# One pair of heads ahead of the others in the first tile of an attention ramp

## The chip, the cores and the metric

The kernel runs on one core of one Trainium2 chip. The metric is the device time of one execution in microseconds, taken as the median of several runs.

## The reference, cut to what matters

Two batches, 8 heads, 768 positions, head size 64. Every query sees 4 sink keys at the start of the sequence and a window of 128 keys; two mixers follow, which hold most of the work and which the change does not touch.

```python
scores = q @ k.transpose(0, 1, 3, 2) / sqrt(64)
keep = (pos[None, :] < 4) | ((rel >= 0) & (rel < 128))   # rel = query - key
a = softmax(where(keep, scores, -1e9))                    # over the keys
x = (a @ v).transpose(0, 2, 1, 3).reshape(2, 768, 512)
# first mixer
u = x + (x^T @ U @ V)^T ; x = u + relu(u @ w_ch1) @ w_ch2
# second mixer, the same with relu between t1 and t2
```

## The kernel before, in words

The core works through one list, `plan`, that every engine walks in the same order; each engine does its own part of each step and waits on semaphores for the others. Attention goes by tiles T of 128 queries and, in each, by heads h; the unit u = 8T + h. For unit u the list holds ("scores", u), ("probsT", u - 2), ("pv", u - 4) for batch 0, and the steps that prepare tile T + 1 stand between them.

What is done to a unit: TensorE makes the scores, in three passes of split numbers (high query by high key, high by low, low by high); VectorE adds the mask and takes the minimum (`masked`, L1172); ScalarE takes the exponential (`probs`, L919); GpSimd copies the probabilities of the sinks into `p_sink` (L853); TensorE transposes the probabilities (L1463), which VectorE (even units) or ScalarE (odd ones) copies to `probs_T` (L1191, L986); TensorE multiplies by v (L1483).

What is done to a tile before its scores: q and k arrive in `q_nat` and `k_nat` (SyncE, `load_qk`, L684 and L686). ("qT", T) and ("kT", T) are four TensorE transposes each, one for every pair of heads (L1430). For T = 0, VectorE makes `q_hi` and `q_lo` from the transposed bank (L1115, L1117), ScalarE the high keys (L959, L960), VectorE the low ones (L574). For T = 1 to 5, ScalarE copies the transposed q and k to SBUF (L944, L953), VectorE casts the high parts (L1126, L1146, L1150) and **GpSimd subtracts for the low parts**: the queries in one step (L563, at "qsplit"), the keys in two, for the even heads (L574, at "ksplit") and for the odd ones (L574, at "ksplit_odd"). Scores 8 (tile 1, head 0) wait for the first of these and scores 9 for the second.

`k_hi` and `k_lo` have three slots of keys for each pair and head of the pair, with the four sink keys behind each slot, and are zeroed at the start: `k_hi` by VectorE (L1089), `k_lo` by GpSimd (L794), each in two steps. GpSimd also makes the identity (L789, L791), zeroes the masks and `sink_raw`, which lies in `o_stage` (L797, L798), and builds four masks with 14 selects (L806), all at its start; masks 2, 3 and then 0 and 1 are used by tiles 0, 1, 2 and 3. SyncE loads the sink values with eight small transfers once `sink_raw` is zeroed, and copies them twice more; VectorE casts them at ("scores", 8) (L1106).

The steps in order for the first units, before: unit 0 is qT(0), kT(0), the splits, qT(1), scores 0; unit 1 scores 1; unit 2 kT(1), qsplit(1), scores 2, probsT 0; unit 3 scores 3, probsT 1; unit 4 scores 4, pv 0, probsT 2; unit 5 ksplit(1), scores 5, pv 1, probsT 3; unit 6 ksplit_odd(1), scores 6 and so on; unit 8 qT(2), scores 8, pv 4, probsT 6; unit 9 scores 9. `keep_busy` issues transposes of the identity into an unused bank (L1415): 8 before qT(0), 6 before qT(1), 2 before scores 0.

Of the kernel before, what the change touches and what calls it, by code (L numbers as in the profile page):

```python
# [5 lines left out]
def attention_then_two_mixers(  # L6
# [58 lines left out]
    def attention(b):  # L65
# [4 lines left out]
        for u in range(lo, hi + LAG_V):  # L70
            T, h = divmod(u, H)
            now, scores, turned, probsT, pv, behind = [], [], [], [], [], []
            if u == 0:
                now += [("qT", T), ("kT", T), ("qsplit", T), ("ksplit", T)]
# [4 lines left out]
            if u < hi and T + 1 < NTILES:  # L79
                (turned if b else now).extend([("qT", T + 1)] if h == 0 else  # L80
                                              [("kT", T + 1), ("qsplit", T + 1)] if h == (2, 3)[b] else [])
                if h == (4 if 0 < T < NQ else 5):
                    (behind if b else now).append(("ksplit", T + 1))
                if h == (6, 7)[b]:
                    now.append(("ksplit_odd", T + 1))
# [96 lines left out]
    BUSY_BEFORE = {("qT", 0): 8, ("qT", 1): 6, ("scores", 0): 2}  # L182
# [132 lines left out]
    with ExitStack() as ctx:  # L315
# [136 lines left out]
        k_first_high = sem("k_first_high")  # L452
        ksinks_high = sem("ksinks_high")
# [82 lines left out]
        def key_parts(k_pad, T):  # L536

            turned = k_full if T else by_pair(tp_banks[tp_bank_of["kT", 0]])
            for e in range(2):
                rows = slice(e * D, (e + 1) * D)  # L540
                src = turned[rows, :, :]
                yield (src, k_pad[rows, :, e, T % 3, 0:P],
# [6 lines left out]
        def queries_split(T):  # L549

            return T + 1 if T < NQ else 2 * (T + 1) - NQ
# [14 lines left out]
        def key_low(eng, wait, T, e):  # L566
# [3 lines left out]
            steps = ((3, 2), (1, 0)) if T == 0 else ((1, 0),)  # L570
            done = (keys_split(T - 1) if T else 0) + e * len(steps)
            for to, of in steps:
                wait(k_split, done)
                eng.tensor_tensor(low[to], low[of], high[to].bitcast(f32), ALU.subtract).then_inc(k_split, 1)  # L574
                done += 1
            wait(k_split, done)

        def keys_split(T):

            return sum(4 if t % NQ == 0 else 2 for t in range(T + 1))  # L580
# [29 lines left out]
        def wait_drained(eng, s):  # L610

            kind, at = s
            if s == ("qT", 0):
                eng.wait_ge(q_split, 1)
# [62 lines left out]
        def _(sp):  # L677
# [43 lines left out]
            load_qk(0)  # L721
# [65 lines left out]
        def _(pool):  # L787
# [5 lines left out]
            for part in (slice(0, 3, 2), slice(1, 2)):  # L793
                nc.gpsimd.memset(k_lo[:, :, :, part, :].rearrange("p a b s k -> p (a b) s k").bitcast(f32), 0.0) \  # L794
                  .then_inc(klo_zeroed, 1)
                if part.start == 0:
                    nc.gpsimd.memset(masks[:, :, :], 0.0).then_inc(masks_built, 1)  # L797
                    nc.gpsimd.memset(sink_raw[0:HS], 0.0).then_inc(vsink_zeroed, 1)  # L798
# [11 lines left out]
            for m, own in MASKS:  # L810
# [9 lines left out]

            split = copied = 0
            for s in plan:
                if s == ("scores", H + 7):
# [81 lines left out]
        def _(act):  # L905
# [20 lines left out]
            for s in plan:  # L926
# [28 lines left out]
                elif s == ("ksplit", 0):  # L955
                    act.wait_ge(khi_zeroed, 2)
                    act.wait_ge(tp_ready, tp_at["kT", 0] + 1)
                    for src, dst, sinks, sink_dst in key_parts(k_hi, 0):
# [128 lines left out]
        def _(dve):  # L1087
            for part in (slice(0, 3, 2), slice(1, 2)):
                nc.vector.memset(k_hi[:, :, :, part, :].rearrange("p a b s k -> p (a b) s k").bitcast(f32), 0.0) \  # L1089
                  .then_inc(khi_zeroed, 1)  # L1090
# [12 lines left out]
            for s in plan:  # L1103
# [8 lines left out]
                if s == ("qsplit", 0):  # L1112
                    turned = by_pair(tp_banks[tp_bank_of["qT", 0]])
                    dve.wait_ge(tp_ready, tp_at["qT", 0] + 1)
                    nc.vector.tensor_scalar(q_hi[:, 0, :, :], turned, -SCALE, None, op0=ALU.mult).then_inc(q_high, 1)  # L1115
                    dve.wait_ge(q_high, 1)
# [579 lines left out]
```

## Time and profile before

| | us |
|---|---|
| median of 3 runs | 623.8 (623.78 to 624.27) |
| profiled execution, its own time | 624.31 |
| its span, first to last instruction | 622.3 |

The profile is of one execution. Times in its rows are microseconds from the start of the span, mean durations are in ns. The engines are PE (TensorE), PEld (its weight loads), DVE (VectorE), ACT (ScalarE), POOL (GpSimd) and SP (SyncE; SPq is its issue of transfers). "out<-in" names what an instruction writes and reads. An "x3" at the end of a row of the timeline means that so many instructions are merged in it. PEclk is the granted clock of TensorE as a share of 2.4 GHz.

### The profile page before, as it was taken

What the parts mean: (1) busy time and instruction counts of PE and PEld (TensorE: products, weight loads), DVE (VectorE), ACT (ScalarE), POOL (GpSimd) and SP (SyncE); (2) the same over time, 40 slices, a digit from 0 to 9 for tenths busy, and PEclk for the clock granted to TensorE, in tenths of its full rate; (3) what the DMA queues carried; (4) which work ended last, traced back from release to release, by engine and by line L of the source; (5) the groups of instructions that cost most, each with busy time, mean ns of one, the idle gap of its engine ahead of it and who ended that gap; (6) DMA issues with size and microseconds to landing.
All of it is one profiled execution on the core that took longest, in us unless ns stands there. A gap on an engine that the chain in (4) does not pass through costs nothing.

```text
span 622.3 us, 10353 instructions
## 1 busy us (share of the span) xinstructions
PE 613.0 (99%) x3462; PEld 554.3 (89%) x3462; DVE 350.1 (56%) x756; ACT 323.0 (52%) x728; POOL 402.5 (65%) x425
## 2 busy tenths in 40 slices
PE   8999999999999999999999999999999999999997
PEld 6899799999999989999999888899998888999986
DVE  6777655464464646866566621685766227665411
ACT  5677665655645555645445344554453437454321
POOL 7776488887978684656656654666575537566352
PEclk9999999999999999999999999999999999999999
DMA  8573345354335334333232333323323433421151
GB/s 162 124 168 82 89 109 131 102 120 120 85 102 168 88 105 132 84 102 86 75 112 86 119 96 100 111 83 93 94 84 119 137 101 85 152 85 41 47 163 72
DMA packets 88467, 65.59 MB, mean 105 GB/s; under 512 B 43040, under 2 KB 72480, under 8 KB 88416
## 3 DMA queue, kind: packets, MB, share of 16 engines
q1 hardware_dynamic: 88416, 64.95, 38.2%
q8 instruction: 28, 0.46, 0.3%
q14 instruction: 23, 0.19, 0.1%
HBM read 61.52 MB, written 3.15 MB: 104 GB/s over the span
## 4 chain that ended last, share of the span: by engine, by line
PE 92%; POOL 2%; DVE 2%; ACT 1%; issue 1%; DMA 1%; SPq 0%; DVEq 0%; ACTq 0%; POOLq 0%
PE bank L1666 34%; PE bank L1407 23%; PE bank L1632 11%; PE bank L1483 5%; PE bank L1453 4%; PE bank L1591 3%; PE bank L1536 3%; PE bank L1463 2%; PE bank L1430 2%; PE bank L1562 1%; POOL w_lo L899 1%; PE bank L1517 1%; PE bank L1658 1%; DMA k_nat<-in_k_dram 1%; DVE b_lo L1276 1%
## 5 line engine op out<-in xcount | busy, mean ns | idle before, releaser
L899 POOL TENSOR_TENSOR w_lo<-w_raw,w_hi 128x512 fp32r<-128x512 f32 (+1 forms) x158 | 210.6, 1340 | 136.0 <-ACT w_hi L935 135.0
L935 ACT ACTIVATE w_hi<-w_raw 128x512 fp32r<-128x512 f32 (+1 forms) x158 | 96.6, 618 | 54.0 <-PE bank L1666 35.9
L1666 PE MATMUL bank<-w_hi,hid_hi 128*128 128x512 f32 x216 | 86.4, 400 | 0.0
L1666 PE MATMUL bank<-w_hi,hid_lo 128*128 128x512 f32 x216 | 85.0, 394 | 0.0
L1666 PE MATMUL bank<-w_lo,hid_hi 128*128 128x512 f32 x216 | 84.8, 393 | 0.0
L919 ACT ACTIVATE probs<-masked,neg_max 128x264 f32<-128x264 f32 (+1 forms) x96 | 47.7, 497 | 59.6 <-DVE neg_max L1172 58.9
L1666 PE MATMUL bank<-w_hi,y_hid 128*128 128x512 f32 x216 | 71.0, 394 | 0.2
L1172 DVE CUSTOM_DVE_ANT_0 masked<-bank,masks 128x264 f32<-128x264 f32 (+1 forms) x96 | 38.8, 405 | 28.0 <-PE bank L1453 25.1
L1483 PE MATMUL bank<-v_nat,probs_T 128*128 128x64 f32 x352 | 50.6, 262 | 0.3 <-ACT probs_T L986 0.2
L1483 PEld LDWEIGHTS bank<-v_nat,probs_T 128*128 128x128 f32 x352 | 47.9, 190 | 1.6 <-ACT probs_T L986 0.9
L1666 PEld LDWEIGHTS bank<-w_hi,y_hid 128*128 128x128 f32 x216 | 40.5, 188 | 9.5 <-POOL w_lo L899 1.5
L1666 PEld LDWEIGHTS bank<-w_hi,hid_lo 128*128 128x128 f32 x216 | 40.5, 188 | 8.9
L1407 PE MATMUL bank<-b_hi,a_hi_even 128*128 128x384 f32 x140 | 47.2, 337 | 0.1
L1407 PE MATMUL bank<-b_hi,a_lo_even 128*128 128x384 f32 x140 | 47.1, 336 | 0.0
L1407 PE MATMUL bank<-b_hi,a_lo_odd 128*128 128x384 f32 x140 | 47.0, 336 | 0.0
L1407 PE MATMUL bank<-b_hi,a_hi_odd 128*128 128x384 f32 x140 | 47.0, 335 | 0.0
L1407 PE MATMUL bank<-b_lo,a_hi_even 128*128 128x384 f32 x140 | 46.9, 335 | 0.0
L1407 PE MATMUL bank<-b_lo,a_hi_odd 128*128 128x384 f32 x140 | 46.9, 335 | 0.0
L1666 PEld LDWEIGHTS bank<-w_lo,hid_hi 128*128 128x128 f32 x216 | 40.7, 188 | 6.7
L1666 PEld LDWEIGHTS bank<-w_hi,hid_hi 128*128 128x128 f32 x216 | 40.7, 189 | 6.6
L1632 PE MATMUL bank<-uT_hi,w_hi 128*128 128x384 f32 x128 | 45.4, 354 | 0.2 <-POOL w_lo L899 0.2
L1632 PE MATMUL bank<-uT_hi,w_lo 128*128 128x384 f32 x128 | 43.2, 338 | 0.0
(181 smaller groups left out, 1495.7 us busy)
## 6 DMA issues: line engine op xcount, KB each, us to landing
w_raw<-in_moe_w_ch_dram SPq DMA_DIRECT2D x144, 256.0 KB, 2.8
w_raw<-in_moe_w_ch_dram SPq DMA_DIRECT2D x20, 512.0 KB, 3.5
q_nat<-in_q_dram SPq DMA_DIRECT2D x12, 256.0 KB, 3.2
k_nat<-in_k_dram SPq DMA_DIRECT2D x12, 256.0 KB, 4.0
v_nat<-in_v_dram SPq DMA_DIRECT2D x12, 256.0 KB, 4.0
out_dram<-o_stage SPq DMA_DIRECT2D x11, 256.0 KB, 3.4
w_raw<-in_moe_w_tok_dram SPq DMA_DIRECT2D x6, 256.0 KB, 2.7
w_raw<-in_moe_w_tok_dram SPq DMA_DIRECT2D x8, 192.0 KB, 2.3
```

The lines of the kernel that those rows point to most:

```text
L899: nc.gpsimd.tensor_tensor(w_lo[:, split % NW, 0:n], w_raw[:, split % NR, 0:n], w_hi[:, split % NW, 0:n].bitcast(f32), ALU.subtract) \
L919: nc.scalar.activation(probs[:, u % 4, 0:n], masked[:, u % 3, 0:n], ACT.Exp, bias=neg_max[:, u % (2 * H):u % (2 * H) + 1], scale=-1.0, acc ...
L935: nc.scalar.activation(w_hi[:, split % NW, 0:n], w_raw[:, split % NR, 0:n], ACT.Copy) \
L1172: nc.vector.tensor_tensor_reduce(out=masked[:, u % 3, 0:n], in0=s_slots(u)[0][:, 0:n], in1=masks[:, mask_of(T), 0:n], scale=1.0, scalar=3. ...
L1407: last = mm(bank[:, 0:HALF], w[at % 2][:, a, k, :], u[:, b_part, k, :], start=(first and n == 0), stop=(n == 5), skip_group_check=True)
L1430: last = nc.tensor.transpose(qk_bank(s)[:, p * P:(p + 1) * P], nat[:, T % 2, p * P:(p + 1) * P], ident[:, :])
L1453: last = mm(bank[:, 0:width(T)], queries, keys(ks, T, h // 2, h % 2), start=(n == 0), stop=(n == len(passes) - 1))
L1483: last = mm(o_bank(T)[:, h * D:(h + 1) * D], probs_T[:, u % 2, j * P:(j + 1) * P], v_nat[:, tile % 3, h * D:(h + 1) * D], start=(h == 0 an ...
L1536: last = mm(m_tile(use)[:, :], w[:, slot, cols], x[:, t % 2, :], start=(t == 0 and n == 0), stop=(t == NQ - 1 and n == 2), skip_group_chec ...
L1591: last = mm(m_tile((s[:4], d))[:, 0:HALF], tok[:, g, rows], w[:, slot, 0:HALF], start=False, stop=(g == KG - 1 and n == 2), skip_group_che ...
L1632: last = mm(m_tile(use)[:, 0:HALF], w[:, slot, rows], u[:, kk, cols], start=(n == 0), stop=(n == 3 * KD - 1))
L1666: last = mm(m_tile(use)[:, :], stationary, w[:, slot, :], start=False, stop=(final and n == 2), skip_group_check=True)
```

## The change

Tile 0 is split into its first pair of heads and the other three. The first pair's q and k (64 KB each) are loaded by transfers of their own, turned by one transpose each into banks of their own (new steps q0T, k0T), and split (q0split, k0split); scores 0 follow. Then come qT(0) for the other three pairs, scores 1, kT(0), qsplit(0) and ksplit(0) for the three pairs, qT(1), scores 2. Scores 0 to 3 each wait for their own part. kT(1) and qsplit(1) stand in unit 3 instead of unit 2. The identity transposes are 5 before q0T, 3 before scores 0 and 4 before qT(1).

The key arrays are zeroed by slot: `k_lo` slot 0 and the sink columns of the other slots first, the rest later on GpSimd; `k_hi` slot 2 goes from VectorE to GpSimd. GpSimd builds only the first mask at its start (4 selects), then zeroes `sink_raw`, then the slots; mask 3 (4 selects) is built at the step ("kT", 1) and masks 0 and 1 (6 selects) at ("scores", 5), ahead of that unit's `p_sink` copy.

```diff
@@ -71,14 +71,17 @@
             if u == 0:
-                now += [("qT", T), ("kT", T), ("qsplit", T), ("ksplit", T)]
+                now += [("q0T",), ("k0T",), ("q0split",), ("k0split",)]
+                behind += [("qT", 0)]
+            elif u == 1:
+                behind += [("kT", 0), ("qsplit", 0), ("ksplit", 0), ("qT", 1)]
             sinks_after = u - (LAG_T if b else LAG_V)
...
             if u < hi and T + 1 < NTILES:
-                (turned if b else now).extend([("qT", T + 1)] if h == 0 else
-                                              [("kT", T + 1), ("qsplit", T + 1)] if h == (2, 3)[b] else [])
+                (turned if b else now).extend([("qT", T + 1)] if h == 0 and u else
+                                              [("kT", T + 1), ("qsplit", T + 1)] if h == (2 if 0 < T < NQ else 3) else [])
                 if h == (4 if 0 < T < NQ else 5):
@@ -179,7 +182,7 @@
-    BUSY_BEFORE = {("qT", 0): 8, ("qT", 1): 6, ("scores", 0): 2}
+    BUSY_BEFORE = {("q0T",): 5, ("scores", 0): 3, ("qT", 1): 4}
     first, second, prepared = attention(0), attention(1), preparation(1, 1)
@@ -533,12 +540,27 @@
-        def key_parts(k_pad, T):
-
-            turned = k_full if T else by_pair(tp_banks[tp_bank_of["kT", 0]])
+        FIRST_BANKS = (banks[7], banks[3])
+        first_pair, other_pairs = slice(0, 1), slice(1, PAIRS)
+
+        def first_key_parts(k_pad, pairs):
+
+            turned = FIRST_BANKS[1][:, 0:P].unsqueeze(1)
+            if pairs is other_pairs:
+                turned = by_pair(tp_banks[tp_bank_of["kT", 0]])[:, pairs, :]
+            count = pairs.stop - pairs.start
             for e in range(2):
...
                 src = turned[rows, :, :]
+                yield (src, k_pad[rows, pairs, e, 0, 0:P],
+                       src[:, :, 0:N_SINK].unsqueeze(2).broadcast_to([D, count, 3, N_SINK]),
+                       k_pad[rows, pairs, e, :, P:BLK])
+
+        def key_parts(k_pad, T):
+
+            for e in range(2):
+                rows = slice(e * D, (e + 1) * D)
+                src = k_full[rows, :, :]
                 yield (src, k_pad[rows, :, e, T % 3, 0:P],
@@ -548,7 +570,7 @@
-            return T + 1 if T < NQ else 2 * (T + 1) - NQ
+            return T + 2 if T < NQ else 2 * (T + 1) - NQ + 1
@@ -567,17 +589,14 @@
             low, high = list(key_parts(k_lo, T))[e], list(key_parts(k_hi, T))[e]
-            steps = ((3, 2), (1, 0)) if T == 0 else ((1, 0),)
-            done = (keys_split(T - 1) if T else 0) + e * len(steps)
-            for to, of in steps:
-                wait(k_split, done)
-                eng.tensor_tensor(low[to], low[of], high[to].bitcast(f32), ALU.subtract).then_inc(k_split, 1)
-                done += 1
+            done = keys_split(T - 1) + e
             wait(k_split, done)
+            eng.tensor_tensor(low[1], low[0], high[1].bitcast(f32), ALU.subtract).then_inc(k_split, 1)
+            wait(k_split, done + 1)
...
-            return sum(4 if t % NQ == 0 else 2 for t in range(T + 1))
+            return sum(8 if t == 0 else 4 if t == NQ else 2 for t in range(T + 1))
@@ -611,7 +630,7 @@
             if s == ("qT", 0):
-                eng.wait_ge(q_split, 1)
+                eng.wait_ge(q_split, queries_split(0))
             elif kind == "qT":
@@ -718,7 +737,12 @@
-            load_qk(0)
+            for nat, x, loaded in ((q_nat, q, first_loaded[0]), (k_nat, k, first_loaded[1])):
+                sp.dma_start(nat[:, 0, 0:P].rearrange("p (h d) -> p h d", h=2), heads(x, 0)[:, 0:2, :]) \
+                  .then_inc(loaded, 16)
+            for nat, x, loaded in ((q_nat, q, q_loaded[0]), (k_nat, k, k_loaded[0])):
+                sp.dma_start(nat[:, 0, P:DM].rearrange("p (h d) -> p h d", h=H - 2), heads(x, 0)[:, 2:H, :]) \
+                  .then_inc(loaded, 16)
             load_v(0)
@@ -790,12 +814,14 @@
                                     base=0, pattern=[[-1, P]], channel_multiplier=1).then_inc(ident_ready, 1)
-            for part in (slice(0, 3, 2), slice(1, 2)):
-                nc.gpsimd.memset(k_lo[:, :, :, part, :].rearrange("p a b s k -> p (a b) s k").bitcast(f32), 0.0) \
-                  .then_inc(klo_zeroed, 1)
-                if part.start == 0:
-                    nc.gpsimd.memset(masks[:, :, :], 0.0).then_inc(masks_built, 1)
-                    nc.gpsimd.memset(sink_raw[0:HS], 0.0).then_inc(vsink_zeroed, 1)
+
+            def zero(k_pad, slots, cols):
+                part = k_pad[:, :, :, slots, cols].rearrange("p a b s k -> p (a b) s k")
+                return nc.gpsimd.memset(part.bitcast(f32), 0.0)
+
+            zero(k_lo, slice(0, 1), slice(0, BLK)).then_inc(klo_zeroed, 1)
+            zero(k_lo, slice(1, 3), slice(P, BLK)).then_inc(klo_zeroed, 1)
+            nc.gpsimd.memset(masks[:, :, :], 0.0).then_inc(masks_built, 1)
             built = 1
@@ -807,7 +833,8 @@
-            for m, own in MASKS:
+            def build(m, own):
+
                 keep(m, own, P, 0, -1, 1)
@@ -818,8 +845,18 @@
+            build(*MASKS[0])
+            nc.gpsimd.memset(sink_raw[0:HS], 0.0).then_inc(vsink_zeroed, 1)
+            for slot in (1, 2):
+                zero(k_lo, slice(slot, slot + 1), slice(0, P)).then_inc(klo_zeroed, 1)
+            zero(k_hi, slice(2, 3), slice(0, P)).then_inc(k_last_zeroed, 1)
             split = copied = 0
             for s in plan:
+                if s == ("kT", 1):
+                    build(*MASKS[1])
+                elif s == ("scores", 5):
+                    for mask in MASKS[2:]:
+                        build(*mask)
                 if s == ("scores", H + 7):
@@ -952,10 +989,14 @@
                                          ACT.Copy).then_inc(k_copied, 1)
-                elif s == ("ksplit", 0):
-                    act.wait_ge(khi_zeroed, 2)
-                    act.wait_ge(tp_ready, tp_at["kT", 0] + 1)
-                    for src, dst, sinks, sink_dst in key_parts(k_hi, 0):
+                elif s in (("k0split",), ("ksplit", 0)):
+                    first = s == ("k0split",)
+                    if first:
+                        act.wait_ge(khi_zeroed, 2)
+                        act.wait_ge(first_turned, 2)
+                    else:
+                        act.wait_ge(tp_ready, tp_at["kT", 0] + 1)
+                    for src, dst, sinks, sink_dst in first_key_parts(k_hi, first_pair if first else other_pairs):
                         nc.scalar.activation(sink_dst, sinks, ACT.Copy)
@@ -1085,9 +1126,9 @@
         def _(dve):
-            for part in (slice(0, 3, 2), slice(1, 2)):
-                nc.vector.memset(k_hi[:, :, :, part, :].rearrange("p a b s k -> p (a b) s k").bitcast(f32), 0.0) \
-                  .then_inc(khi_zeroed, 1)
+            for slots, cols in ((slice(0, 1), slice(0, BLK)), (slice(1, 3), slice(P, BLK)), (slice(1, 2), slice(0, P))):
+                part = k_hi[:, :, :, slots, cols].rearrange("p a b s k -> p (a b) s k")
+                nc.vector.memset(part.bitcast(f32), 0.0).then_inc(khi_zeroed, 1)
@@ -1109,13 +1150,17 @@
                                             ALU.subtract).then_inc(vsink_split, 1)
-                if s == ("qsplit", 0):
-                    turned = by_pair(tp_banks[tp_bank_of["qT", 0]])
-                    dve.wait_ge(tp_ready, tp_at["qT", 0] + 1)
-                    nc.vector.tensor_scalar(q_hi[:, 0, :, :], turned, -SCALE, None, op0=ALU.mult).then_inc(q_high, 1)
-                    dve.wait_ge(q_high, 1)
-                    nc.vector.scalar_tensor_tensor(out=q_lo[:, 0, :, :], in0=turned, scalar=-SCALE,
-                                                   in1=q_hi[:, 0, :, :].bitcast(f32),
+                if s in (("q0split",), ("qsplit", 0)):
+                    if s == ("q0split",):
+                        pairs, turned, done = first_pair, FIRST_BANKS[0][:, 0:P].unsqueeze(1), q_first_high
+                        dve.wait_ge(first_turned, 1)
+                    else:
+                        pairs, turned, done = other_pairs, by_pair(tp_banks[tp_bank_of["qT", 0]])[:, 1:, :], q_high
+                        dve.wait_ge(tp_ready, tp_at["qT", 0] + 1)
+                    nc.vector.tensor_scalar(q_hi[:, 0, pairs, :], turned, -SCALE, None, op0=ALU.mult).then_inc(done, 1)
+                    dve.wait_ge(done, 1)
+                    nc.vector.scalar_tensor_tensor(out=q_lo[:, 0, pairs, :], in0=turned, scalar=-SCALE,
+                                                   in1=q_hi[:, 0, pairs, :].bitcast(f32),
                                                    op0=ALU.mult, op1=ALU.subtract).then_inc(q_split, 1)
@@ -1129,17 +1174,22 @@
                         moved.then_inc(q_moved, 1)
-                elif s == ("ksplit", 0):
+                elif s in (("k0split",), ("ksplit", 0)):
+                    pairs, made = (first_pair, 0) if s == ("k0split",) else (other_pairs, 2)
                     dve.wait_ge(klo_zeroed, 2)
-                    for e in range(2):
-                        dve.wait_ge(k_first_high, e + 1)
-                        key_low(nc.vector, lambda sem, n: None, 0, e)
+                    for e, (low, high) in enumerate(zip(first_key_parts(k_lo, pairs), first_key_parts(k_hi, pairs))):
+                        dve.wait_ge(k_first_high, made + e + 1)
+                        for to, of in ((3, 2), (1, 0)):
+                            nc.vector.tensor_tensor(low[to], low[of], high[to].bitcast(f32),
+                                                    ALU.subtract).then_inc(k_split, 1)
                 elif s[0] == "ksplit":
...
                     if T == 1:
-                        dve.wait_ge(khi_zeroed, 2)
+                        dve.wait_ge(khi_zeroed, 3)
+                    if T == 2:
+                        dve.wait_ge(k_last_zeroed, 1)
                     if T >= 2:
@@ -1418,7 +1468,12 @@
                     keep_busy(BUSY_BEFORE[s])
-                if s[0] in ("qT", "kT"):
+                if s in (("q0T",), ("k0T",)):
+                    n = int(s == ("k0T",))
+                    pe.wait_ge(first_loaded[n], 16)
+                    nc.tensor.transpose(FIRST_BANKS[n][:, 0:P], (q_nat, k_nat)[n][:, 0, 0:P], ident[:, :]) \
+                      .then_inc(first_turned, 1)
+                elif s[0] in ("qT", "kT"):
                     T = s[1]
@@ -1426,19 +1481,22 @@
                         tp_free(s)
-                    for p in range(PAIRS):
+                    for p in range(0 if T else 1, PAIRS):
                         last = nc.tensor.transpose(qk_bank(s)[:, p * P:(p + 1) * P],
...
                     T, h = divmod(u, H)
-                    if h == 0:
+                    if T == 0 and h < 4:
+                        pe.wait_ge(q_split, h // 2 + 1)
+                        pe.wait_ge(k_split, 2 * (h + 1))
+                    elif h == 0:
                         pe.wait_ge(q_split, queries_split(T))
...
                             pe.wait_ge(k_moved, T - NQ + 2)
-                        pe.wait_ge(k_split, keys_split(T) - (2 if T == 0 else 0 if T == NQ else 1))
+                        pe.wait_ge(k_split, keys_split(T) - (0 if T == NQ else 1))
                     elif h == 1:
```

## Rows read from the trace of the kernel before

**Rows 1.** The page's busy time: us (share of the span) xinstructions.

```profile
PE 613.0 (99%) x3462; PEld 554.3 (89%) x3462; DVE 350.1 (56%) x756; ACT 323.0 (52%) x728; POOL 402.5 (65%) x425
```

**Rows 2.** Two stretches: length, each engine's busy us (x instructions), PEclk, DMA share, GB/s.

```profile
16.00:17.00 1.00, 0.27 (x3) 0.08 (x2) 0.74 (x1) 0.09 (x1) 0.94 (x2) 1.00 0.71 127
20.00:40.00 20.00, 20.00 (x166) 18.33 (x165) 14.20 (x52) 14.50 (x50) 14.87 (x29) 1.00 0.66 152
```

**Rows 3.** Timeline, TensorE at scores 9: start, us, engine, line, operation [idle before <-releaser].

```profile
16.93 0.39 PE L1453 MATMUL bank<-k_hi,q_hi 128*128 128x264 f32 x1 [0.73 <-POOL k_lo L574]
```

**Rows 4.** Timeline, GpSimd up to tile 1's low keys, with a cast of VectorE.

```profile
10.86 0.19 POOL L853 COPY p_sink<-probs 128x12 f32<-128x12 f32 x1 [1.61 <-ACT probs L919]
11.24 0.19 POOL L853 COPY p_sink<-probs 128x12 f32<-128x12 f32 x1 [0.19 <-ACT probs L919]
11.59 1.28 POOL L563 TENSOR_TENSOR q_both<-uT_full,q_hi 128x512 fp32r<-128x512 f32 x1 [0.16 <-POOL p_sink L853]
12.82 0.32 POOL L853 COPY p_sink<-probs 128x12 f32<-128x12 f32 x2
13.33 0.20 POOL L853 COPY p_sink<-probs 128x12 f32<-128x12 f32 x1 [0.19 <-ACT probs L919]
13.66 0.42 DVE L1150 CAST k_hi<-uT_full 64x512 fp32r<-64x512 f32 x1
13.66 1.55 POOL L574 TENSOR_TENSOR k_lo<-uT_full,k_hi 64x512 fp32r<-64x512 f32 x1
...
15.60 1.27 POOL L574 TENSOR_TENSOR k_lo<-uT_full,k_hi 64x512 fp32r<-64x512 f32 x1
```

**Rows 5.** Timeline, VectorE at the sink values and score 8.

```profile
16.26 0.90 DVE L1106 CAST v_sink<-o_stage 96x512 fp32r<-96x512 f32 x1 [1.43 <-DMA o_stage<-o_stage]
...
17.08 0.42 DVE L1172 CUSTOM_DVE_ANT_0 masked<-bank,masks 128x264 f32<-128x264 f32 x1
```

**Rows 6.** Timeline, VectorE up to the first x_nat, TensorE behind it.

```profile
20.41 0.28 DVE L1195 TENSOR_TENSOR p_sinkT<-bank,p_sinkT 32x128 fp32r<-32x128 f32 x1 [0.50 <-ACT p_sinkT L995]
...
22.92 0.69 DVE L1207 TENSOR_TENSOR x_nat<-bank,recip 128x512 f32<-128x512 f32 x1
...
23.84 1.02 PE L1517 MATMUL bank<-x_nat,U_sb 128*96 128x512 f32 x2
```

**Rows 7.** Timeline, SyncE's issues and GpSimd's zeroing in the opening.

```profile
3.93 1.40 SPq L686 DMA_DIRECT2D k_nat<-in_k_dram  x1
...
4.20 0.94 POOL L798 MEMSET o_stage<- 32x1024 f32 x1
5.09 0.97 POOL L794 MEMSET k_lo<- 128x1056 f32 x1
...
5.37 3.53 SPq L726 DMA_DIRECT2D o_stage<-in_v_dram  x8
```

**Rows 8.** Timeline, tile 0's keys, tile 1's queries, the first scores and masking.

```profile
5.73 1.12 PE L1430 MATMUL bank<-ident,k_nat 128*128 128x128 f32 x4 [0.43 <-DMA k_nat<-in_k_dram]
...
7.05 0.58 ACT L960 ACTIVATE k_hi<-bank 64x512 fp32r<-64x512 f32 x1
...
7.74 1.65 DVE L574 TENSOR_TENSOR k_lo<-bank,k_hi 64x48 fp32r<-64x48 f32 x4 [0.99 <-ACT k_hi L960]
...
8.13 1.11 PE L1430 MATMUL bank<-ident,q_nat 128*128 128x128 f32 x4
...
9.28 0.31 PE L1453 MATMUL bank<-k_hi,q_hi 128*128 128x132 f32 x1
...
9.96 0.30 DVE L1172 CUSTOM_DVE_ANT_0 masked<-bank,masks 128x132 f32<-128x132 f32 x1 [0.57 <-PE bank L1453]
```

**Rows 9.** Timeline, the mask selects: all fourteen, then the last six.

```profile
6.03 3.23 POOL L806 TENSOR_SCALAR_AFFINE_SELECT masks<-masks 128x128 f32<-128x128 f32 x14
...
7.94 1.31 POOL L806 TENSOR_SCALAR_AFFINE_SELECT masks<-masks 128x128 f32<-128x128 f32 x6
```

**Rows 10.** Timeline, four transposes later on, at 25.69.

```profile
25.69 0.60 PE L1430 MATMUL bank<-ident,q_nat 128*128 128x128 f32 x4
```

More of the change, by code:

```diff
@@ L452, in attention_then_two_mixers @@
         k_first_high = sem("k_first_high")
+        first_loaded = [sem("q_first_loaded"), sem("k_first_loaded")]
+        first_turned = sem("first_turned")
+        q_first_high = sem("q_first_high")
+        k_last_zeroed = sem("k_last_zeroed")
         ksinks_high = sem("ksinks_high")
```

## The prediction

> **What bounds the kernel now.** I read the page first: TensorE has work in 613.0 us, 99% of the span [rows 1]. Time can be gained or lost only where TensorE stands, or where a stall of it grows. The table of stretches shows where it stands early: it is busy for 0.27 us between 16 and 17 us, and for all 20.00 us between 20 and 40 [rows 2]. So the opening, up to about 17 us, is a ramp that ends with a stall, and after it TensorE is packed.
>
> Then I asked what ends that stall. The TensorE rows show scores(9) starting at 16.93 after a wait for GpSimd's k_lo [rows 3]: score 9 is the first odd head of tile 1, and its wait is for both halves of tile 1's low keys. GpSimd's own rows show why these are late [rows 4]: p_sink copies of scores 0 and 1 at 10.86 and 11.24, the low queries at 11.59, three more copies, low keys at 13.66 and, behind one more copy, low keys again at 15.60. From 11.24 on it hardly rests. GpSimd's in-order queue is the ramp's critical path.
>
> One more engine is nearly as late. VectorE waits 1.43 us for the copied sink values and casts them at 16.26, and masks score 8 only behind that, at 17.08 [rows 5]. From there it works almost without rest to x_nat's end at 23.61, and TensorE takes that up at 23.84 [rows 6]. So even if GpSimd were early, little could be won: the VectorE chain leaves what it can itself absorb, its one idle of 0.50 us at 20.41 [rows 6].
>
> **The change, part by part.** *Loads.* SyncE issues four loads for q and k of tile 0 in place of two, the bytes being the same. The issue for k of tile 1, the fifth, took 1.40 us, where eight small ones took 3.53 together [rows 7]: it looks held back by the data in flight, and two more short ones at the front should cost little; I take q of tile 1 to land where it did, 8.1, and at most 0.4 us later. Behind them on SyncE are the eight sink loads. They began at 5.37, and wait for GpSimd's zeroing of o_stage, which ended at 5.14 [rows 7]. In the new order GpSimd does k_lo's slot 0 (1056 elements, 0.97), 64 elements of sinks (0.1 to 0.2), masks (the same size, the same time), four mask selects (0.95, below) and then o_stage (0.94) [rows 7]: begun at 1.5, behind the identity, that ends at 5.5 to 5.6. The sink values then land about 0.3 us later, so VectorE's cast starts at about 16.5 and scores 8 is masked at 17.4. That costs nothing as long as TensorE starts score 9 after about 17.3; if GpSimd's chain were gone, it would be the bound.
>
> *Zeroing.* VectorE has one slot of k_hi less to zero, which goes to GpSimd, and is done before the first turned queries come. GpSimd's three slot memsets (about 0.95 each, by the 0.97 of the nearest size [rows 7]) now lie from 5.6 to 8.45. They are hidden: its next work that anything waits for is p_sink(2), at 11. Only 2 us of this cover are left.
>
> *The first pair.* Its q and k can be in at about 3.3 and 3.7. Two slow transposes, ScalarE's two high parts and VectorE's low parts put scores(0) near 5.1, four microseconds before 9.28 [rows 8]. But scores 2 lies behind the first turn of tile 1's queries, qT(1). Its four transposes began at 8.13 when the data came, and the scores followed at 9.28 [rows 8]. Nor can k's other pairs be much earlier: they are turned after scores 1, near 7.0 to 7.9 (data at 5.73 before), ScalarE splits them behind probabilities(1) until 9.3 (its copy of four pairs took 0.58 us, of three some 0.47, with a short one of 0.1 ahead, twice), and VectorE ends its low parts near 10.1 (four steps in 1.65 before, 1.4 now) [rows 8]. Scores 2 starts near 9.5 and masking 2 at 10.1. From masking 0 at 9.96 to its p_sink copy at 10.86 were 0.90 us [rows 4, 8]; the same step puts p_sink(2) at 11.0. My bounds for it are 10.7 and 11.4. Two of eight heads are early, but GpSimd's q and k work of tile 1, which was the critical path, starts behind p_sink(2) now: the turn of k(1) and the query split moved from unit 2 to unit 3.
>
> *The masks put off.* Before, all 14 selects ran from 6.03 to 9.26 while GpSimd had nothing else to do; it then stood idle for 1.61 us [rows 4, 9]. Now four of them stand at kT(1), just before the low queries, and six at scores(5), between the two halves of the low keys. The last six took 1.31 us and the first eight 1.9, so four cost about 0.95 [rows 9]. Both lots are now on the chain that releases score 9, and nothing on TensorE's side fills the time. This is the term that decides.
>
> **The sum**, from p_sink(2)'s start to scores(9): the copy 0.20; four selects 0.95; handoff 0.10; low queries to the next copy 1.23; second copy 0.12; to the low keys 0.33; low keys 1.30; six selects 1.33; copy and handoff 0.33; low keys and handoff 1.32 [rows 3, 4, 9]. That is 7.21 us. Added to 11.0 it is 18.2, against 16.93: 1.3 us later. One cost is open: the first low-key step took 1.55 us and the second 1.27 [rows 4], and the first began with VectorE's cast at 13.66, 0.42 long [rows 4]. I add half of that 0.27, and keep 0 and 0.54 as ends. This makes 1.4 us.
>
> A rule bears on that last term: by the Trainium skill, page "SBUF — State Buffer", section "SBUF: two separate sides", VectorE and GpSimd lock a shared port pair and the loser is blocked for the whole instruction. By it each meeting would cost up to the cast's 0.42 us and not 0.27, so 0.15 us more; this trace shows the smaller price.
>
> After score 9 nothing gives the time back, as TensorE was packed there and does the same steps in the same order. At most the few gaps between 17 and 20 us close, 0.1 us; with the rest of the rounding I leave 1.4. The profiled execution took 624.31 us, its span and 2.0 around it, and would take 625.7; the median of the runs is 0.5 below it, so I predict 625.2.
>
> **Rivals.** (a) *The shift is there but small*, 0.3 to 1.2 us: p_sink(2) comes at 10.7, no port meeting, and selects that follow each other faster. For it: my time for p_sink(2) has many steps. Against it: the selects alone are 2.3 us, and the copy that the low queries stand behind starts only from 11.24 (p_sink(1) then) to 11.0 (p_sink(2) now) earlier. Time 624.6.
>
> (b) *No stall is lengthened, the kernel gets a little faster*: if p_sink(2) started before 9.7 us, 7.21 us would end before 16.93. For it: scores 0 and 1 are four microseconds early. Against it: qT(1) stands ahead of scores 2 and its data came at 8.13. Its price is small, since VectorE's wait for the sinks stays: 0.15 to 0.5 us, 623.4. A gain above 1.25 us would need the sink values early too, of which I see nothing.
>
> (c) *TensorE's clock falls.* The table grants 1.00 (the 2.4 GHz level) everywhere, but four transposes took 1.11 us at 8.13 and 0.60 us at 25.69 [rows 8, 10], so the opening ran at half rate in spite of it. Scores 8 would start at 15.3 (11.0 and the first seven terms, 4.23), TensorE's work behind it lasts 0.9 us, so it would stand for about 2 us before score 9, where it stood 0.73 before [rows 3]. If it restarts at half rate, half of the slow stretch is lost; for an estimated 2 to 7 us of it (the opening's four transposes were slow at 5.73 and still at 8.13) that adds 1 to 3.5 us, 2 in the middle: time 627.2. Against it: once fast, TensorE stayed fast over the stall of 0.73 us. The Trainium skill, page "TensorE: Matmul & The Clock Gate", section "Part 1: The HAM clock gate", says that activity releases the throttle and idleness brings it back; by it the gap works for this rival, and no row of this trace shows a fall.
>
> (d) *Both later starts and port meetings*: p_sink(2) at 11.4 and 0.54 of meetings give 2.2 us, 626.0; an end of my forecast, not a case of its own.
>
> **How the numbers follow.** A measurement of this kernel tells about 0.2%, 1.25 us, from no change. The forecast (0.9 to 2.2 us later, bounds from the two open costs) has 0.70, (a) 0.13, (b) 0.09, (c) 0.08. The forecast crosses the line of 1.25 us: of its 0.70 I give 0.22 to below it. Slower: 0.48 and all of (c), 0.56. Within: 0.22, all of (a), and 0.05 of (b) at its price, 0.40. Faster: the other 0.04 of (b), where the sinks would be early as well. The range, 624.3 to 626.6, takes the forecast, most of (a) and the low end of (c); (b) and the rest, about 0.18, are left out.
>
> **What the new profile would show.** Right: scores(0) near 5.1; scores(2) at 9.3 to 9.7; four selects after p_sink(2) and six between the two k_lo steps, the second ending near 18.2; TensorE idle for about 2 us before scores(9) at 18.2 to 18.6, released by GpSimd's k_lo; VectorE's v_sink cast near 16.5. Wrong: scores(9) before 17, the selects finished before p_sink(2), or a wait for another engine there. The weakest steps are the start of p_sink(2) and whether TensorE's rate holds.

## The result, and the profile after

The changed kernel takes 627.38 us (median of 5 runs, 626.76 to 628.57) against 623.8 of the kernel before: a ratio of 1.0059, 95% interval 1.0048 to 1.0071. It is slower, as forecast, but by 3.6 us where 1.4 was forecast, and above the range. The profiled execution took 627.02 us with a span of 625.3, 3.0 over the span before.

The stretches of the profile after (length, busy us of each engine, PEclk, DMA share, GB/s) answer to [rows 2]:

```profile
16.00:19.00 3.00, 0.76 (x6) 0.57 (x6) 0.93 (x4) 1.26 (x4) 2.85 (x8) 1.00 0.86 185
20.00:24.00 4.00, 4.00 (x23) 3.77 (x22) 3.10 (x11) 2.82 (x11) 1.85 (x4) 0.57 0.57 127
```

Two things are to be seen. TensorE works for 0.76 of the three microseconds up to 19, while GpSimd works for 2.85. And behind the stall the granted clock is 0.57 for four microseconds; finer stretches show 0.50 (the 1.2 GHz level) from about 20.5 to 23.9.

TensorE's timeline around scores 9 answers to [rows 3], and its first "down" (the product of x_nat with U, in the first mixer) to [rows 6]:

```profile
16.31 0.33 PE L1541 MATMUL bank<-v_nat,probs_T 128*128 128x64 f32 x2
16.48 0.28 PE L1521 MATMUL bank<-ident,probs 128*128 128x128 f32 x1
19.04 0.39 PE L1511 MATMUL bank<-k_hi,q_hi 128*128 128x264 f32 x1 [2.28 <-POOL k_lo L594]
...
26.73 1.07 PE L1575 MATMUL bank<-x_nat,U_sb 128*96 128x512 f32 x2
```

Scores 9 start 2.11 us later than before (19.04 against 16.93), for GpSimd's low keys as before; the first "down" is 2.89 us later (26.73 against 23.84). So 2.1 us of the 3.0 are lost at the stall, 0.8 in the slow stretch behind it, and 0.1 later. The medians lie 3.6 us apart and the profiled executions 2.7 (627.02 and 624.31), so the shares are read off an execution that lost somewhat less than the median one.

GpSimd's timeline, which answers to [rows 4], with VectorE's casts of the even and the odd high keys:

```profile
11.31 0.19 POOL L890 COPY p_sink<-probs 128x12 f32<-128x12 f32 x1 [2.87 <-ACT probs L956]
...
11.45 1.01 POOL L832 TENSOR_SCALAR_AFFINE_SELECT masks<-masks 128x128 f32<-128x128 f32 x4
...
12.42 1.27 POOL L585 TENSOR_TENSOR q_both<-uT_full,q_hi 128x512 fp32r<-128x512 f32 x1
...
12.57 1.40 DVE L1196 CAST k_hi<-uT_full 64x512 fp32r<-64x512 f32 x1
...
13.64 0.52 POOL L890 COPY p_sink<-probs 128x12 f32<-128x12 f32 x2
...
14.22 0.42 DVE L1200 CAST k_hi<-uT_full 64x512 fp32r<-64x512 f32 x1
14.29 1.48 POOL L594 TENSOR_TENSOR k_lo<-uT_full,k_hi 64x512 fp32r<-64x512 f32 x1
...
15.92 1.53 POOL L832 TENSOR_SCALAR_AFFINE_SELECT masks<-masks 128x128 f32<-128x128 f32 x6
...
17.73 1.26 POOL L594 TENSOR_TENSOR k_lo<-uT_full,k_hi 64x512 fp32r<-64x512 f32 x1
```

Both lots of selects stand in the chain, 1.01 and 1.53 us, and GpSimd had stood idle for 2.87 us just ahead of it. The opening went nearly as the steps of the prediction said (these rows answer to [rows 5, 8]):

```profile
5.07 0.45 PE L1511 MATMUL bank<-k_hi,q_hi 128*128 128x132 f32 x1 [0.41 <-DVE k_lo L1183]
...
8.70 1.09 PE L1485 MATMUL bank<-ident,q_nat 128*128 128x128 f32 x4
...
9.51 0.45 PE L1511 MATMUL bank<-k_hi,q_hi 128*128 128x132 f32 x1
...
9.97 0.40 PE L1511 MATMUL bank<-k_hi,q_both 128*128 128x132 f32 x1
...
10.41 0.29 DVE L1222 CUSTOM_DVE_ANT_0 masked<-bank,masks 128x132 f32<-128x132 f32 x1 [0.34 <-PE bank L1511]
...
15.86 0.42 DVE L1147 CAST v_sink<-o_stage 96x512 fp32r<-96x512 f32 x1 [0.47 <-DMA o_stage<-o_stage]
```

Scores 0 are at 5.07 in place of 9.28, and scores 2 at 9.51. Tile 1's queries came at 8.70 in place of 8.13.

### The profile page after: what moved, and what is told of

Its sections match the earlier page's. It is cut to its first block, busy times and chain, and to the rows that moved or that the text cites. A ratio compares the mean times of both kernels' runs of the same rounds, so it can differ in the third digit from the quotient of the medians.

```text
span 625.3 us, 10364 instructions
## 1 busy us (share of the span) xinstructions
PE 614.5 (98%) x3458; PEld 555.5 (89%) x3458; DVE 350.8 (56%) x763; ACT 324.0 (52%) x732; POOL 403.2 (64%) x428
## 4 chain that ended last, share of the span: by engine, by line
PE 91%; POOL 2%; DVE 2%; ACT 1%; issue 1%; DVEq 0%; ACTq 0%; POOLq 0%
PE bank L1724 34%; PE bank L1457 23%; PE bank L1690 11%; PE bank L1541 5%; PE bank L1511 4%; PE bank L1649 3%; PE bank L1594 3%; PE bank L1521 2%; PE bank L1620 1%; PE bank L1485 1%; POOL w_lo L936 1%; PE bank L1575 1%; PE bank L1716 1%; DVE b_lo L1326 1%; PE bank L1642 0%
```

## The experiments

The theory tested (A) is that the put-off selects on GpSimd's queue make the loss and that TensorE's clock falls because of the stall. Its rivals: the later place of kT(1) and the meetings of VectorE with GpSimd (B), and a fall of the clock with another cause (C). Each ratio is to the kernel before as timed on the same chip: 624.15 us for the first four kernels, 624.34 for "only the six early" and for the last kernel, 623.92 for the three between. "The stall" is TensorE's wait just ahead of scores 9. A table at the end of this section has all kernels side by side.

**All masks early.** In the changed kernel:

```diff
+            for mask in MASKS[1:]:
+                build(*mask)
             split = copied = 0
             for s in plan:
-                if s == ("kT", 1):
-                    build(*MASKS[1])
-                elif s == ("scores", 5):
-                    for mask in MASKS[2:]:
-                        build(*mask)
```

> The changed kernel with all ten put-off selects built right behind the slot memsets, ahead of the list. Theory A (the selects on GpSimd's queue are the loss, the clock's fall follows from the stall): the selects end before p_sink(2) at 11.3, scores 9 start at 19.04 less 1.1 and 1.65, near 16.3, the granted clock stays 1.00, the time is 623.3, 4 us under the changed kernel. Rival B (the loss is the later place of kT(1) and the query split, and the meetings of VectorE's casts with GpSimd): scores 9 stay behind 17.5 and the time is 624.5 or more.

Measured: 624.03 us, ratio 0.9999 (0.9991 to 1.0008), granted clock 0.999 to 1.00 in all 11 runs. The whole loss is gone with the ten selects, though kT(1) still stands in unit 3: its later place alone costs nothing that can be measured (rival B's first half). But scores 9 start at 16.98 and not 16.3:

```profile
10.34 0.32 POOL L887 COPY p_sink<-probs 128x12 f32<-128x12 f32 x2
11.33 0.19 POOL L887 COPY p_sink<-probs 128x12 f32<-128x12 f32 x1 [0.68 <-ACT probs L953]
11.68 1.27 POOL L585 TENSOR_TENSOR q_both<-uT_full,q_hi 128x512 fp32r<-128x512 f32 x1 [0.15 <-POOL p_sink L887]
...
15.66 1.26 POOL L594 TENSOR_TENSOR k_lo<-uT_full,k_hi 64x512 fp32r<-64x512 f32 x1
```

The selects end before p_sink(2), and from there the chain is that of the kernel before, started at the same time: 11.33 to 16.98 here, 11.24 to 16.93 there [rows 3, 4]. The first pair's four microseconds are worth nothing at scores 9, because the low queries stand behind p_sink(2) where they stood behind p_sink(1).

**Only the four early.** The build of mask 3 ahead of the list, the six at scores(5) as in the changed kernel.

> Only the four selects of mask 3 are built early, the six stay between the two halves of the low keys. Theory A: scores 9 at 17.9 to 18.0, TensorE stands 1.2 to 2 us, time 624.9 if the clock holds and 625.8 if it falls. Rival B: little change against the changed kernel, 627.

Measured: 625.99 us, ratio 1.0025 (1.0015 to 1.0036). Scores 9 at 17.94, as expected, but scores 8 moved forward too (14.81), so the stall is 2.25 us:

```profile
15.41 0.28 PE L1520 MATMUL bank<-ident,probs 128*128 128x128 f32 x1
17.94 0.39 PE L1510 MATMUL bank<-k_hi,q_hi 128*128 128x264 f32 x1 [2.25 <-POOL k_lo L594]
```

The seven runs fall into two sorts: four with a mean clock of 0.996 or 0.997 at 625.99 to 626.33, and three with 1.00 at 625.16 to 625.55. The same program thus shows the fall's price with nothing else changed: 626.02 less 625.51, the medians of the two sorts, 0.5 us (the openings may differ too, as only one run was profiled).

**TensorE kept busy in the stall.** In the changed kernel:

```diff
-    BUSY_BEFORE = {("q0T",): 5, ("scores", 0): 3, ("qT", 1): 4}
+    BUSY_BEFORE = {("q0T",): 5, ("scores", 0): 3, ("qT", 1): 4, ("scores", 9): 18}
```

> The changed kernel with 18 identity transposes ahead of scores 9, inside the stall, nothing else. Theory A: the clock fell because TensorE stood 2.3 us; filled, it is granted 1.00 throughout, scores 9 still start at 19.0, and the time falls by 0.8 to 1.7 us to 625.7 to 626.6. Rival C (the clock falls for another reason, such as the opening's changed load, or is no part of the loss): clock 0.997 or time 627.4 as before.

Measured: 626.27 us (626.20 to 626.89), ratio 1.0036 (1.0022 to 1.0050), clock 0.999 or 1.00 in all five runs:

```profile
16.61 2.13 PE L1465 MATMUL bank<-ident 128*128 128x128 f32 x18
19.04 0.39 PE L1511 MATMUL bank<-k_hi,q_hi 128*128 128x264 f32 x1 [0.30 <-POOL k_lo L594]
...
25.94 1.02 PE L1575 MATMUL bank<-x_nat,U_sb 128*96 128x512 f32 x2
```

Scores 9 start at the same 19.04, and the first "down" comes 6.90 us behind them, as in the kernel before (6.91) and not 7.69 as in the changed kernel: 0.8 us are the price of the fall in the profiled executions (0.7 by the two spans, 625.3 and 624.6). By the medians it is 1.1 us (627.38 less 626.27), or 1.5 when each is taken against the kernel before on its own chip (3.6 less 2.1). Rival C is out: filled with transposes that compute nothing of use, the stall no longer brings the clock down. The 2.1 us that remain (626.27 less 624.15) are the stall itself, 19.04 less 16.93.

**Only the masks put off, in the kernel before.** No first pair, the loads and the zeroing as they were; the selects as in the change.

```diff
+            build(*MASKS[0])
             split = copied = 0
             for s in plan:
+                if s == ("kT", 1):
+                    build(*MASKS[1])
+                elif s == ("scores", 5):
+                    for mask in MASKS[2:]:
+                        build(*mask)
```

> The kernel before with only the masks put off: four selects at kT(1), six at scores 5, all else as it was. Theory A: scores 9 move from 16.93 to about 19.4 (1.0 and 1.5 us), the stall reaches 3 us, the clock falls, time 626.2 without the fall and 627.1 with it. Rival B: the selects fall in gaps of GpSimd between the p_sink copies and the time is under 624.5.

Measured: 626.77 us, ratio 1.0041 (1.0029 to 1.0054), clock 0.997 in all five runs. This one edit makes 2.6 of the 3.6 us. The other 1.0 isn't the rest of the change by itself, which costs nothing with all masks early; the spans differ by 0.8 us, and the earlier opening of this execution (below) can make that up. Whether it makes up the medians' 1.0 isn't shown. Scores 9 are at 18.17 and not 19.4. Part of the gap is the opening, which is 0.9 us earlier in this execution, p_sink(0) at 9.99 for 10.86 before:

```profile
7.66 0.77 PE L1437 MATMUL bank<-ident,q_nat 128*128 128x128 f32 x4
```

The four transposes of tile 1's queries begin at 7.66 and take 0.77 us, where they took 1.11 at 8.13 before. The last kernel below, a kernel before with all selects at the start, shows the same early opening (7.76 and 0.73), so this isn't the edit's doing and differs between executions. Counted from the second p_sink copy, scores 9 come after 7.72 us here (10.45 to 18.17) and after 5.69 before (11.24 to 16.93): 2.0 us longer, where 2.5 were expected and the selects ran 1.02 and 1.50 us. About half a microsecond of them cost nothing: it lay where GpSimd had small gaps before, and the first low keys took 1.35 us for 1.55. The stall is 2.26 us and the clock is granted 0.54 in the two microseconds up to 20:

```profile
18.17 0.59 PE L1460 MATMUL bank<-k_hi,q_hi 128*128 128x264 f32 x1 [2.26 <-POOL k_lo L574]
```

```profile
16.00:18.00 2.00, 0.00 (x0) 0.00 (x0) 0.58 (x4) 0.61 (x2) 1.86 (x5) 1.00 1.06 239
18.00:20.00 2.00, 1.83 (x9) 1.83 (x10) 0.77 (x3) 0.29 (x1) 0.58 (x4) 0.54 0.07 13
```

**Only the six early.** The order of MASKS becomes 2, 0, 1, 3; mask 3 is built at kT(1), the others ahead of the list.

> The mirror of e3_four_early: the six selects early, only mask 3's four at kT(1) (the order in which the masks count changes with it, their content doesn't). Theory A: scores 9 at 17.3 to 17.5, and scores 8 as in the changed kernel at 15.9, so TensorE stands 0.6 to 0.9 us between them, the granted clock stays 1.00 in every run and the time is 624.2 to 624.8. If the clock's fall doesn't come from the stall, some runs fall to 0.997 and lie 0.7 us above the others.

Measured: 625.13 us, ratio 1.0015 (1.0004 to 1.0027). Scores 9 at 17.68 with 0.81 us of wait. Nine of eleven runs have a clock of 0.999 or 1.00 and lie at 624.5 to 625.3; two fell to 0.997 and lie at 626.2 and 626.5. I had expected no fall in any. In the profiled run, which kept its clock, TensorE stands twice, 0.87 us for probs_T at 15.05 and 0.81 at 17.68. Whether two such waits brought the clock down in the other two, or a longer one, isn't shown, as neither was profiled.

**Four selects behind the low queries.** In the changed kernel, `("kT", 1)` in GpSimd's loop becomes `("ksplit", 1)`.

> The changed kernel with the four selects of mask 3 moved from ahead of the low queries to ahead of the first low keys. VectorE's cast of the even high keys then no longer runs into the low queries at 12.57, where it took 1.40 us. Theory A (only the length of GpSimd's queue counts): scores 9 stay at 18.8 to 19.1, TensorE's wait of 0.85 us for probs_T at 14.9 is gone or smaller, the clock falls as before, and the time is 627.0 to 627.6. Rival B (the meeting holds up the chain): scores 9 come 0.6 us or more earlier and the time is 626.5 or less.

Measured: 627.14 us, ratio 1.0057 (1.0045 to 1.0069), clock 0.994 to 0.997. Scores 9 at 18.89, 0.15 us earlier, and all of that is p_sink(2), at 11.16 for 11.31: from there to scores 9 it is 7.73 us in both. VectorE's cast takes 0.50 us and not 1.40, and TensorE's 0.85 us for probs_T is gone; it only waits that much longer elsewhere (0.7 more before scores 8). The meeting of the two engines is real and isn't what sets the end: rival B's second half is out.

**kT(1) back in unit 2.** All masks early, and `(2 if 0 < T < NQ else 3)` is `(2, 3)[b]` again.

> All masks early, as in e1_masks_early, and kT(1) and the query split back in unit 2. Theory A, with what e1_masks_early showed (GpSimd's chain from p_sink(2) at 11.33 to scores 9 at 16.98): the low queries come ahead of p_sink(2), but q_copied is there only at 10.5, so the chain starts at about 11.0 and gains 0.2 to 0.6 us; scores 9 at 16.4 to 16.8, time 623.5 to 624.0. Rival B (the later place of kT(1) was a loss of its own): scores 9 below 16.2, time below 623.3. Rival D: kT(1) ahead of scores 2 waits for its data, masked 2 comes later and nothing is gained, 624.0 to 624.6.

Measured: 626.51 us over 12 runs, in two sorts: five at 623.98 to 624.76 and seven at 626.35 to 627.45, all with a granted clock of 0.999 or 1.00. The profiled run is of the second sort:

```profile
16.01 0.63 PE L1538 MATMUL bank<-v_nat,probs_T 128*128 128x64 f32 x2
...
17.81 1.06 PE L1482 MATMUL bank<-ident,q_nat 128*128 128x128 f32 x4
...
20.99 0.60 PE L1482 MATMUL bank<-ident,k_nat 128*128 128x128 f32 x4
```

Four transposes take 1.06 us at 17.81 and 0.60 at 20.99: the slow rate of the opening lasted until about 20.8 here, where it ended near 9.2 before. In the faster sort nothing is gained over the kernel before (623.92), which agrees with all masks early: the place of kT(1) was no loss of the change. The kernel before has one such run too, 627.16 us at a clock of 1.00 among its 21 on the last chip, so the slower sort doesn't belong to this order alone. Why the slow rate lasts in this order stays open; in its opening TensorE waited 0.7 us for the first pair's keys and twice 0.4 for low keys, small gaps in a stretch that was busy otherwise.

**Even low keys by VectorE.** First on top of all masks early, with the sink values taken up at scores 9 and 11:

> All masks early, as in e1_masks_early; VectorE makes the even low keys of tile 1 (0.7 us) in place of GpSimd (1.4 us), and takes up the sink values at scores 9 and 11 in place of 8 and 10. Theory A (GpSimd's queue sets scores 9, and VectorE's sink values are the next bound): scores 9 at 15.4 to 15.8 against 16.98, the stall there gone, time 623.0 to 623.5, 0.6 to 1.1 us under e1_masks_early. Rival E (VectorE, with 0.7 us more, becomes the bound at once): TensorE waits for probs_T or masked instead and the time is 623.8 or more.

Measured: 624.5 us, ratio 1.0008 (0.9999 to 1.0016). Scores 9 start at 16.86, and nothing is won: TensorE waits 0.82 us for probs_T at 15.36, later for probs_T and v_sink (0.32 and 0.27). Part of the 16.86 is a late opening in this execution (scores 0 at 5.82 for 5.08 with all masks early), so the place of scores 9 decides little; the time and the new waits are what rival E said. Then on the kernel before alone, GpSimd's step and VectorE's:

```diff
-                elif s[0] in ("ksplit", "ksplit_odd") and s[1]:
+                elif s[0] in ("ksplit", "ksplit_odd") and s[1] and s != ("ksplit", 1):
...
                         last = nc.vector.tensor_copy(dst, src)
                     last.then_inc(k_high, 1)
+                    if T == 1:
+                        dve.wait_ge(k_high, keys_high(1, 0))
+                        key_low(nc.vector, lambda sem, n: None, 1, 0)
```

> The kernel before, with the even low keys of tile 1 made by VectorE and nothing else changed. If the GpSimd queue was the ramp's bound with room behind it: scores 9 at 15.9 to 16.3, time 623.2 to 623.6. Rival E (VectorE's added 0.7 us and its sink values take its place, as in e8_even_by_vector): TensorE waits for probs_T or later for VectorE, time 623.7 to 624.4.

Measured: 623.7 us against 624.34, ratio 0.9992 (0.9983 to 1.0001). Scores 9 are at 15.91, one microsecond earlier, but 0.7 to 0.8 of it is this execution's earlier opening (second p_sink copy at 10.56 for 11.24, scores 0 at 8.47 for 9.28); of the edit's own there may be 0.3 us. VectorE's step takes 0.68 us for GpSimd's 1.27 to 1.55. It is the fastest kernel of the study by its median, but its interval reaches no change: a gain is not shown.

**All kernels side by side.** Times in us, the last four columns of the profiled execution. "Stall" is TensorE's wait at scores 9, "other" its longest wait between 12 us and scores 9, "to down" the time from scores 9 to the first "down".

| kernel | ratio | runs under 0.999 | scores 9 | stall | other | to down |
|---|---|---|---|---|---|---|
| before | 1 | none | 16.93 | 0.73 | none | 6.91 |
| changed | 1.0059 | 5 of 5 | 19.04 | 2.28 | 0.85 | 7.69 |
| all masks early | 0.9999 | 0 of 11 | 16.98 | 0.72 | none | 6.92 |
| only the four early | 1.0025 | 4 of 7 | 17.94 | 2.25 | none | 7.65 |
| changed, kept busy | 1.0036 | 0 of 5 | 19.04 | 0.30 | 0.77 | 6.90 |
| before, masks put off | 1.0041 | 5 of 5 | 18.17 | 2.26 | 0.62 | 7.82 |
| only the six early | 1.0015 | 2 of 11 | 17.68 | 0.81 | 0.87 | 6.90 |
| four behind the low queries | 1.0057 | 5 of 5 | 18.89 | 2.25 | 0.68 | 7.62 |
| kT(1) in unit 2 | 1.0028 | 0 of 12 | 19.72 | none | none | 7.28 |
| masks early, even low keys by VectorE | 1.0008 | 0 of 11 | 16.86 | none | 0.82 | 7.55 |
| before, even low keys by VectorE | 0.9992 | 0 of 11 | 15.91 | none | 0.84 | 6.92 |

The last column gives the fall's price four times over: 7.62 to 7.82 us where the profiled run fell, 6.90 to 6.92 where it kept its clock and nothing else held TensorE up (7.28 is the kernel with the slow rate up to 20.8, 7.55 the one that waits for probs_T and v_sink). From the first "down" to the end of the span it is 598.5 to 598.7 us in all eleven, so whatever the profiled executions lose or win is decided before it.

## Why the prediction was right in direction and wrong in size

- **What bounds the ramp** (GpSimd's in-order queue, by TensorE's wait at scores 9): right for the changed kernel. Taking the selects out of it took the loss away. In the kernel before, easing that queue by one step gave no gain that is shown (0.9992, interval to 1.0001), as the prediction's paragraph on VectorE had it.
- **The masks put off, "the term that decides"**: right, and shown from both sides. Without them the loss is gone (0.9999); alone in the kernel before they make 1.0041.
- **The first pair**: right; scores 0 at 5.07 for 5.1, scores 2 at 9.51 for 9.5, and no gain from them where it counts. p_sink(2) came at 11.31 for 11.0. The data of q(1) were late, 8.70 for 8.13 to 8.5, but scores 2 started on time in spite of it; their three passes still ran at the slow rate, 0.86 us from 9.51 where scores 0 took 0.52 from 9.28 before, and so masking 2 began at 10.41 for 10.1.
- **The sum**: it came to 18.35 with half a meeting; measured were 19.04. The terms, measured and forecast: p_sink(2) 11.31 for 11.0; copy, four selects and handoff 1.11 for 1.25; low queries to the next copy 1.22 for 1.23; two copies to the low keys 0.65 for 0.45; low keys to the selects 1.63 for 1.44; six selects to the copy 1.48 for 1.33; the last two 0.33 and 1.31 for 0.33 and 1.32. The differences add to 0.69 us, none of them above 0.31. The stall's 2.1 us lay inside the bounds (up to 2.2), so up to here the range would have held.
- **The step that failed is the clock: rival (c) kept apart from the sum.** The sum said that TensorE would stand for about 2 us, and yet took the work behind score 9 at full rate ("nothing gives the time back", 0.1 us of closing gaps); the fall of the clock was priced as a thing apart, with a chance of 0.08. All five runs of the changed kernel show it (0.997 in three, 0.994 in two). Forecast and rival should have been one case.
- **What it cost instead.** In the profiled execution the fall is 3.4 us at 0.50 and costs 0.8 us between scores 9 and the first "down": 1.4 + 0.7 for the longer chain + 0.8 makes 2.9 of the 3.0 us by which the spans differ. With the 1.5 us that the filled stall gives back by the medians it makes the 3.6. The rest of that price is open: the two runs with 0.994 lie at 628.55 and 628.57, 1.5 us above the median of the other three, 627.02, and neither was profiled.
- **The price inside rival (c)** was too high. It took half of the slow stretch, 1 to 3.5 us, 2 in the middle, so its 627.2 lies near the measured 627.38 partly by luck: it had too small a stall (1.4 us against 2.1) and too dear a fall. The length of the slow stretch was inside the 2 to 7 us. Gaps of TensorE took up a little of it (behind scores 9 it was busy 6.65 of 6.90 us with the stall filled and all of 7.69 with the fall); why no more than 0.8 us were lost stays open.
- **The rule that stood with rival (c)** is the Trainium skill's, page "TensorE: Matmul & The Clock Gate", section "Part 1: The HAM clock gate": idleness brings the throttle back. The trace agrees, 1.00 before a stall of 2.28 us and 0.50 from 1.4 us behind its end, and the filled stall, with 1.00 throughout, shows the cause.
- **The port meetings**: on GpSimd's chain the row's price held. The low keys took 1.48 us beside a cast that had begun 0.07 us before them and 1.26 alone, 0.22 more, for the 0.27 of the row. What the sum didn't have is the other side: VectorE's cast took 1.40 us for 0.42, as it began at 12.57, inside the low queries (12.42 to 13.69), and ended at 13.97. It cost VectorE, and not the chain that mattered.
- **The rule on that**: by the Trainium skill, page "SBUF — State Buffer", section "SBUF: two separate sides", the one that comes second is blocked for the whole instruction of the first. For VectorE's cast the trace nearly agrees, 0.98 us longer with 1.12 us of the low queries still to run; for GpSimd's low keys it shows 0.22 us, with 0.35 us of the cast still to run.
- **The sink values** landed earlier and not later (15.86 for 16.26 before, 16.5 forecast). The eight small loads began 0.5 us later, at 5.88, but took 2.99 us to issue for 3.53. Nothing hung on it.
- **Rivals (a) and (b)** (a small loss, and none) fell: p_sink(2) would have had to start at 10.7 and before 9.7, and started at 11.31.

## What to carry to other kernels

Work that was done early on an idle engine isn't free to move later: look where the idle time of its in-order queue lies (here 2.9 us just ahead of the chain) and what stands behind the new place. When a sum says that TensorE will stand for some two microseconds, the price of a fall of its clock (0.7 to 0.9 us in the four profiles here) belongs in the same sum, and filling the stall with transposes that nothing needs is a cheap test of it.

## What the runs showed of the hardware that I had not expected

- A stall of TensorE of 2.25 to 2.28 us in the profiled execution went with a mean granted clock of 0.994 to 0.997 in all fifteen runs of three kernels (the changed one, the masks alone, the four selects behind the low queries). Each of these has another wait of 0.62 to 0.85 us, which ended less than 2 us ahead of it; a fourth kernel has the 2.25 us alone, and fell in four of seven runs. Where the longest wait there was 0.72 to 0.84 us, no run fell (the kernel before, all masks early, and both kernels with the low keys on VectorE); where it had two, 0.87 and 0.81 us, two of eleven runs fell. That the shorter wait adds to the long one is not tested apart.
- The rate at the start isn't in the granted clock: the windows give 1.00 while four transposes take 1.06 to 1.12 us in place of 0.60 to 0.63. The end of that stretch moved between executions, from inside the four transposes at 7.66 to about 9.2 us before, about 10.1 in the changed kernel, and 20.8 in one kernel, whose two sorts of runs lie some 2.5 us apart with the same granted clock. A time read off one execution's opening is good to about 0.9 us only, and the same holds for the start of scores 9.
- A VectorE cast of 0.42 us stretched to 1.40 beside a GpSimd subtraction that had begun 0.15 us before it. Where the cast began first, by 0.07 us, it kept its 0.42, and the subtraction took 1.48 us for 1.26.
